# A lag of three pairs in the second MLP: three buffers for h, and both second products of a pair behind seven block products in one go

## The reference, cut to what matters

```python
x = moe_ref(attention(q, k, v))                    # 4608 x 512
h = x @ w_in                                       # 512 -> 1024
e = np.exp(h - h.max(-1)); sm = e / (e.sum(-1) + 1e-9)
solu = h * sm
mu = solu.mean(-1); var = ((solu - mu) ** 2).mean(-1)
ln = (solu - mu) / np.sqrt(var + 1e-6) * g_ln
out = ln @ w_out                                   # 1024 -> 512
```

## Time and profile before

| | |
|---|---|
| time before, median of 3 runs | 1238.48 us (1237.42 to 1242.6) |
| the profiled execution's own time | 1237.77 us |
| its span, first to last instruction | 1236.0 us |
| mean granted TensorE clock | 0.988 |
| PE, DVE, ACT, POOL busy | 97%, 74%, 43%, 25% |
| first block product of the second MLP | starts at 832.63 us |
| copy of the last output tile (ACT, L1163) | starts at 1232.00 us |

### The profile page before, as it was taken

One profiled execution on the slowest core, in us unless ns is written; L12 is line 12 of the kernel. 1 busy time (PEld: TensorE's weight loads), 2 busy tenths in 40 slices (PEclk: granted clock), 3 DMA queues, 4 the chain that ended last, 5 costly groups with the idle time before them and its releaser, 6 DMA issues.

```text
span 1236.0 us, 16164 instructions
## 1 busy us (share of the span) xinstructions
PE 1196.8 (97%) x6013; PEld 988.3 (80%) x6013; DVE 909.0 (74%) x1165; ACT 537.1 (43%) x744; POOL 310.0 (25%) x233
## 2 busy tenths in 40 slices
PE   7999999999999999999999999997889999999997
PEld 6778887878788888888888888985667888888886
DVE  7869678686773577869777686754789888888872
ACT  4443434434353334444434444333454554545441
POOL 5632413224141000000000000124543545353400
PEclk9999999999999999999999999998899999999999
DMA  9797787878865654270642704693355454544333
GB/s 229 226 283 261 238 258 232 249 249 261 268 191 181 236 198 172 74 237 35 196 145 85 238 17 161 207 293 105 125 166 171 150 156 155 152 159 151 135 128 111
DMA packets 211918, 225.07 MB, mean 182 GB/s; under 512 B 63208, under 2 KB 148224, under 8 KB 211712
## 3 DMA queue, kind: packets, MB, share of 16 engines
q1 hardware_dynamic: 206064, 212.50, 54.7%
q0 software_dynamic: 5728, 11.53, 3.3%
q10 hardware_dynamic: 48, 0.01, 0.0%
HBM read 128.51 MB, written 95.48 MB: 181 GB/s over the span
## 4 chain that ended last, share of the span: by engine, by line
PE 77%; DVE 8%; DMA 4%; issue 4%; POOL 2%; SPq 2%; ACT 2%; POOLq 0%; DVEq 0%; ACTq 0%
PE ps_y L1840 8%; PE ps_y L1842 7%; PE ps_y L1841 7%; PE ps_y L1926 5%; PE ps_y L1928 5%; PE ps_y L1930 5%; PE ps_y L1984 5%; PE ps_y L1985 5%; PE ps_y L1986 5%; PE ps_m L1926 3%; PE ps_m L1928 3%; PE ps_m L1930 2%; PE ps_m L1965 2%; PE ps_m L1969 2%; PE ps_m L1967 2%
## 5 line engine op out<-in xcount | busy, mean ns | idle before, releaser
L1840 PE MATMUL ps_y<-X,W 128*128 128x512 f32 x576 | 226.7, 394 | 0.0
L1842 PE MATMUL ps_y<-X,W 128*128 128x512 f32 x576 | 224.4, 390 | 0.0
L1841 PE MATMUL ps_y<-X,W 128*128 128x512 f32 x576 | 224.3, 389 | 0.0
L1364 DVE SCALAR_TENSOR_TENSOR gst<-gst,nslope,ps_y 128x512 f32<-128x512 f32 x144 | 104.4, 732 | 111.0 <-ACT gst L967 110.6
L967 ACT ACTIVATE gst<-ps_y 128x512 f32<-128x512 f32 x144 | 85.7, 596 | 224.8 <-PE ps_y L1842 166.1
L836 POOL TENSOR_TENSOR x2r<-x2r 128x256 f32<-128x256 f32 x18 | 25.1, 1394 | 410.0 <-DMA x2r<-x_scratch 410.0
L1984 PE MATMUL ps_y<-WO,zh 128*128 128x512 f32 x288 | 115.3, 400 | 11.9 <-DVE zl L1665 11.9
L1840 PEld LDWEIGHTS ps_y<-X,W 128*128 128x128 f32 x576 | 108.1, 188 | 23.1
L1842 PEld LDWEIGHTS ps_y<-X,W 128*128 128x128 f32 x576 | 108.1, 188 | 22.8
L1841 PEld LDWEIGHTS ps_y<-X,W 128*128 128x128 f32 x576 | 108.1, 188 | 22.0
L1926 PE MATMUL ps_y<-rh,WOc 128*128 128x512 f32 (+1 forms) x320 | 118.6, 371 | 3.0 <-DVE rl L1526 2.9
(11 more groups left out here) (189 smaller groups left out, 2519.5 us busy)
## 6 DMA issues: line engine op xcount, KB each, us to landing
g_scratch<-gst SPq DMA_DIRECT2D x144, 256.0 KB, 3.5
RX<-g_scratch SPq DMA_DIRECT2D x36, 512.0 KB, 3.6
z_scratch<-zb SPq DMA_DIRECT2D x36, 512.0 KB, 2.7
zt<-z_scratch SPq DMA_DIRECT2D x144, 128.0 KB, 2.9
ws_scratch<-whl SPq DMA_DIRECT2D x22, 512.0 KB, 4.5
RY<-g_scratch SPq DMA_DIRECT2D x18, 512.0 KB, 4.0
RZ<-g_scratch SPq DMA_DIRECT2D x18, 512.0 KB, 4.6
x2r<-x_scratch SPq DMA_DIRECT2D x18, 512.0 KB, 5.0
```

The lines of the kernel that those rows point to most:

```text
L1364: nc.vector.scalar_tensor_tensor(gst[:, n % 3, :], gst[:, n % 3, :], nslope[:, f:f + 1], ps_y[:, f % 4, :], ALU.mult, ALU.add).then_inc(g_ ...
L1840: nc.tensor.matmul(o, W1[:, f, 0, a, :], x[:, 0, a, :], start=(a == 0), stop=False)
L1841: nc.tensor.matmul(o, W1[:, f, 0, a, :], x[:, 1, a, :], start=False, stop=False)
L1842: mm = nc.tensor.matmul(o, W1[:, f, 1, a, :], x[:, 0, a, :], start=False, stop=(a == KT - 1))
```

## The change

PE now does, for pair n, k = 0, 1, 2, 3, 4, 6, 5 in one go and then both tiles of pair n-3. h gets a third buffer. The orders of DVE, ACT, POOL and SP are rewritten to fit. In the last (small) double chunk of the stage before, the units use three buffers instead of two, `x2_high(0)` comes two products earlier, `x2_high(1)` goes between the last two units, `load_x2(1)` is issued earlier (its place in memory is swapped with that of a low part), and DVE does its two posts before the low part of unit (4, 1). The computation is the same. In the two long loops of ACT and DVE below, the conditions that leave out pairs before 0 and behind 17 are not printed.

```diff
-        hs = ((h00, h01), (h10, h11t))
+        hs = ((h00, h01), (h10, h11t), (h20, h21))
...
-                self.slot = 1 + s % 2 if self.single else r % 3
-                if self.single:
-                    self.before = r - 2 if s >= 2 else r - 3
-                else:
-                    self.before = r - 3
+                self.slot = r % 3
+                self.before = r - 3
...
+                if u == PAIRS:                      # SP
+                    sp.wait_ge(bl_ok, number(PAIRS, 3, 1) + 1)
+                    load_x2(1)
                 store_x2(u, 3, p1, c22_ok, 2 * (u + 1), y22_st)
...
+            for n in range(5, PERIODS + 4):         # SP
+                if n - 4 < PERIODS:
+                    store_out(n - 4, 1)
+                if n - 2 < PERIODS:
+                    store_z(n - 2, 0)
+                    load_z(n - 2, 0)
+                if n - 3 < PERIODS:
+                    store_out(n - 3, 0)
+                if n - 2 < PERIODS:
+                    store_z(n - 2, 1)
+                    load_z(n - 2, 1)
                 if n + 3 < PERIODS:
                     load_x2(n + 3)
...
             x2_low(0)                               # POOL
+            x2_sums(1)
             load_wo2(0)
             load_wo2(1)
-            x2_sums(1)
             x2_low(1)
             x2_sums(2)
             x2_low(2)
+            x2_sums(3)
             power(0, 0)
-            x2_sums(3)
             x2_low(3)
+            x2_sums(4)
             power(0, 1)
-            x2_sums(4)
+            x2_low(4)
+            x2_sums(5)
             power(1, 0)
-            x2_low(4)
             power(1, 1)
-            x2_sums(5)
+            x2_low(5)
+            x2_sums(6)
             power(2, 0)
             power(2, 1)
...
+            for n in range(5, PERIODS + 2):
+                power(n - 2, 0)
+                power(n - 2, 1)
                 if n + 1 < PERIODS:
                     x2_low(n + 1)
                 if n + 2 < PERIODS:
                     x2_sums(n + 2)
...
-                    if t.u == LAST_U and t.k == 4:  # ACT, in the units
+                    if t.u == LAST_U and t.k == 2:
                         x2_high(0)
+                if t.u == LAST_U and t.k == 6 and t.j == 0:
+                    x2_high(1)
...
+            for n in range(5, PERIODS + 4):         # ACT; each call only where its pair exists
+                square_tile(n - 2, 1)
+                first_copy(n)
+                out_copy(n - 4, 1)
+                zt_high(n - 3, 1)
+                x2_high(n + 1)
+                out_copy(n - 3, 0)
+                h11_copy(n)
+                zt_high(n - 2, 0)
+                exp_tile(n - 1, 0)
+                exp_tile(n - 1, 1)
+                square_tile(n - 1, 0)
...
+                if t.u == LAST_U and t.k == 4:      # DVE, in the units
+                    if t.j == 0:
+                        post("v", t.u)
+                        post("c22", t.u)
+                    continue
+                if t.u == LAST_U and t.k == 5:
+                    b_turn(UNITS[number(t.u, 4, t.j)])
...
             tile_solu(0, 0)                         # DVE, the single calls
             form_early(1)
+            norm_tile(0, 0)
+            form_21(1)
+            form_12(1)
+            form_early(2)
             tile_solu(0, 1)
...
+            for n in range(5, PERIODS + 3):         # DVE; each call only where its pair exists
+                zt_low(n - 3, 0)
+                form_early(n)
+                form_21(n)
+                form_12(n)
+                norm_tile(n - 2, 0)
+                zt_low(n - 3, 1)
+                norm_tile(n - 2, 1)
+                tile_max(n - 1, 0)
+                tile_max(n - 1, 1)
+                tile_solu(n - 1, 0)
+                tile_solu(n - 1, 1)
...
             for n in range(PERIODS):                # PE
-                for k in range(4):
+                for k in (0, 1, 2, 3, 4, 6, 5):
                     m1_product(n, k)
                 if n >= 3:
+                    m2_product(n - 3, 0)
                     m2_product(n - 3, 1)
-                for k in range(4, PARTS):
-                    m1_product(n, k)
-                if n >= 2:
-                    m2_product(n - 2, 0)
-            m2_product(PERIODS - 3, 1)
-            for n in range(PERIODS - 2, PERIODS):
+            for n in range(PERIODS - 3, PERIODS):
                 for t in range(2):
                     m2_product(n, t)
```

More of the change, by code:

```diff
@@ L713, in _ @@
             load_z(0, 1)
+            load_x2(6)
             store_out(0, 0)
@@ L718, in _ @@
             load_z(1, 1)
-            load_x2(6)
+            load_x2(7)
             store_out(0, 1)
@@ L1168, in _ @@
             exp_tile(0, 0)
+            x2_high(2)
             first_copy(1)
             exp_tile(0, 1)
-            x2_high(2)
             square_tile(0, 0)
             h11_copy(1)
-            square_tile(0, 1)
+            x2_high(3)
             first_copy(2)
-            x2_high(3)
-            exp_tile(1, 0)
             h11_copy(2)
             zt_high(0, 0)
+            square_tile(0, 1)
+            first_copy(3)
+            x2_high(4)
+            exp_tile(1, 0)
             exp_tile(1, 1)
+            zt_high(0, 1)
@@ L1181, in _ @@
             square_tile(1, 0)
-            zt_high(0, 1)
             square_tile(1, 1)
-            first_copy(3)
+            h11_copy(3)
             out_copy(0, 0)
-            x2_high(4)
+            x2_high(5)
             exp_tile(2, 0)
+            first_copy(4)
+            zt_high(1, 0)
             exp_tile(2, 1)
-            zt_high(1, 0)
             out_copy(0, 1)
             square_tile(2, 0)
-            h11_copy(3)
+            zt_high(1, 1)
             square_tile(2, 1)
-            zt_high(1, 1)
+            out_copy(1, 0)
@@ L1195, in _ @@
+            h11_copy(4)
             exp_tile(3, 0)
-            first_copy(4)
-            out_copy(1, 0)
             exp_tile(3, 1)
-            x2_high(5)
+            zt_high(2, 0)
             square_tile(3, 0)
[L1201 to L1213, removed]
+            for n in range(5, PERIODS + 4):
+                if n - 2 < PERIODS:
+                    square_tile(n - 2, 1)
+                if n < PERIODS:
+                    first_copy(n)
+                if n - 4 < PERIODS:
+                    out_copy(n - 4, 1)
+                if n - 3 < PERIODS:
+                    zt_high(n - 3, 1)
@@ L1673, in _ @@
             form_early(0)
+            form_21(0)
             form_12(0)
             tile_max(0, 0)
-            form_21(0)
             tile_max(0, 1)
@@ L1679, in _ @@
             form_early(1)
+            norm_tile(0, 0)
+            form_21(1)
+            form_12(1)
+            form_early(2)
             tile_solu(0, 1)
-            form_12(1)
-            form_21(1)
-            norm_tile(0, 0)
+            zt_low(0, 0)
+            form_21(2)
+            form_12(2)
+            norm_tile(0, 1)
+            form_early(3)
             tile_max(1, 0)
-            form_early(2)
-            norm_tile(0, 1)
-            zt_low(0, 0)
             tile_max(1, 1)
@@ L1689, in _ @@
             tile_solu(1, 0)
-            form_12(2)
-            form_21(2)
             tile_solu(1, 1)
+            zt_low(0, 1)
+            norm_tile(1, 0)
+            form_21(3)
+            form_12(3)
+            norm_tile(1, 1)
             tile_max(2, 0)
             tile_max(2, 1)
-            zt_low(0, 1)
-            norm_tile(1, 0)
-            form_early(3)
-            norm_tile(1, 1)
             tile_solu(2, 0)
             zt_low(1, 0)
+            form_early(4)
             tile_solu(2, 1)
-            form_12(3)
@@ L1703, in _ @@
-            form_21(3)
-            tile_max(3, 0)
             norm_tile(2, 0)
-            tile_max(3, 1)
             norm_tile(2, 1)
             zt_low(1, 1)
+            form_21(4)
+            form_12(4)
+            tile_max(3, 0)
+            tile_max(3, 1)
             tile_solu(3, 0)
-            form_early(4)
             tile_solu(3, 1)
-            norm_tile(3, 0)
-            zt_low(2, 0)
-            form_12(4)
-            form_21(4)
-            tile_max(4, 0)
-            norm_tile(3, 1)
@@ L1718, in _ @@
-            zt_low(2, 1)
-            tile_max(4, 1)
-            tile_solu(4, 0)
-            tile_solu(4, 1)
-            for n in range(5, PERIODS):
-                norm_tile(n - 1, 0)
-                norm_tile(n - 1, 1)
-                form_early(n)
-                zt_low(n - 2, 0)
-                zt_low(n - 2, 1)
-                form_12(n)
-                tile_max(n, 0)
-                form_21(n)
-                tile_max(n, 1)
-                tile_solu(n, 0)
-                tile_solu(n, 1)
@@ L1734, in _ @@
-            n = PERIODS - 1
-            norm_tile(n, 0)
-            norm_tile(n, 1)
-            for t in range(2):
-                zt_low(n - 1, t)
-            for t in range(2):
-                zt_low(n, t)
```

(17 more changed lines are left out.)

109 lines of the change are left out of this document (31 added, 78 removed).

## The result

Predicted were 1277 us (1253 to 1290), with 0.89 for slower. The changed kernel takes a median of 1283.14 us (1278.21 to 1286.8, 4 executions) beside 1237.95 us (1235.4 to 1242.6, 4 executions) for the kernel before: ratio 1.0358, 95% interval 1.0307 to 1.0409. The profiled execution is the fastest of the four, 1278.21 us with a span of 1276.4 us. One execution, of 3055.63 us in experiment 2, was disturbed and is left out of every median and ratio. Every kernel in this study does the whole computation.

What follows compares the result with a forecast made beforehand. The prediction took PE at full clock to bound the middle, with time to win only at the ends. Its terms 926.2 + 286.8 + 57.8 + 4.3 gave a span of 1275.1, forecast 1277.5 us, range 1253 to 1290.

Steps and rivals of the forecast that it cites:

- first block product: Start of the second MLP, where the units end: forecast 833.2 us, against 832.6 before, with some 3.6 idle.
- start of pair 5: Forecast 916.7 us, from work and 14.1 us of stalls in the first pairs; a gain of 13.
- twelve periods: Middle, pair 5 to pair 17: 23.9 us per pair, 286.8 in all (276 to 296); PE alone 244.8.
- the end, up to PE's last matmul: Eight tiles after the last block product: 43.5 us plus waits for low parts and clock, 57.8 (48 to 62).
- Chain A: Middle: POOL's x2_low holds DVE's norm, 3.75 us lost per pair; first_copy late, PE idles 2.6 us per pair.
- X: Moment PE ends the seven products of pair n; first_copy(n+1) is due 16.3 us later.
- R1: Rival: Chain A doesn't happen, Chain B does; period 22.2 to 22.7 us, 1256 us, with clock up to 1265; chance 0.20.
- Chain B: Middle, on ACT: exp stands behind zt_high, which waits for a tile's way through DRAM; late by 1.8 to 2.3 us.
- R2: Rival: neither chain late, PE stays the bound; 1232 us, or 1223 with a shorter end; chance 0.11.
- The clock: PE's clock falling behind gaps, 1.7 us lost each; in the middle taken for half of the pairs.
- from the execution to the median: Last step of the sum: 0.7 us added, as the median before was above its profiled execution; 1276.9 to 1277.5.
- The stalls up to pair 5 and at the end: Idle in units 3.6, pair 2 5.2, pair 4 2.4 and 1.9, tile (1, 1) 0.7; end 6.6 and 3.3 us.

Runs made afterwards that it cites:

- experiment 2: Changed kernel with both exp ahead of zt_high(n-2, 0) on ACT: 1274.18 us, ratio 1.0287 against the kernel before.
- experiment 1: Changed kernel with POOL's x2_low(n) waiting until both tiles of pair n-3 are past the norm: 1283.24 us, ratio 1.0365 against the kernel before.
- experiment 3: Changed kernel with both edits, x2_low waiting for the norm and exp ahead of zt_high: 1231.93 us, ratio 0.995 against the kernel before.
- experiment 4: Changed kernel with exp ahead of zt_high and, from pair 6, POOL's x2_low cut into two 128x896 instructions: 1247.03 us, ratio 1.0066.
- experiment 7: Kernel of experiment 6 with zt_low(n, 0) of pairs 15 and 16 between the two solu of the pair behind: 1233.78 us, ratio 0.9962.
- experiment 6: Kernel of experiment 3 with norm_tile(0, 0) moved behind form_21(1) and form_12(1) on DVE: 1234.58 us, ratio 0.9974 against the kernel before.
- experiment 5: Kernel before with only the units' part of the change, second MLP as before: 1228.89 us, ratio 0.9923.

## Why the prediction was right

Its sum, term by term, against the profiled execution of the changed kernel:

| term | predicted | measured |
|---|---|---|
| first block product | 833.2 | 833.56 |
| start of pair 5 | 916.7 | 916.66 |
| end of its block products | 926.2 | 916.66 + 42 x 0.2267 = 926.2 |
| twelve periods | 286.8 | 1213.09 - 926.2 = 286.9 |
| the end, up to PE's last matmul | 57.8 | 1272.26 - 1213.09 = 59.2 |
| last output | 4.3 | 1276.4 - 1272.26 = 4.1 |
| span | 1275.1 | 1276.4 |

PE's last matmul starts at 1272.03; with the 0.23 us that one takes from start to start, that is 1272.26.

The first row is close partly by luck. Six more profiled executions have the same code up to there; in those of experiments 1 to 4 and 7 the first block product starts at 834.37 to 836.65, in that of experiment 6, behind one more stall, at 840.22.

**Chain A** was the chain that decides. Predicted: L1656 (L1639 now) at 4.3 to 4.6 us in some 13 instructions, POOL 0.06 ahead of it, the copy at X + 18.9, gaps of 2.6. Measured: 4.53, 13, 0.07, X + 19.0, 2.73. Experiment 4 shows the cause by its size, and experiments 2 and 3 by its presence. Rival R1's mechanism is out: POOL was first in all 13 meetings, by 0.06 to 0.07 us. The Trainium skill (SBUF — State Buffer, section "SBUF: two separate sides") has the lock held for the whole instruction; experiment 4 agrees, 2.60 us behind half of POOL's instruction and 4.53 behind all of it.

**Chain B** was there, covered by A. Experiment 1 uncovers it with 2.11 us, of which some 0.3 is a solu that met POOL's sums (1.60 instead of 1.28). Its middle is R1's case too, and R1 was priced too low: it gave 22.4 us a period and 1256 in all, and the twelve periods of experiment 1 take 1217.0 - 929.2 = 287.8, which is 24.0 each. That sum left out the edge of each gap and the clock. So the time could not have told A from B; the held norm and the length of the gap did.

**R2** asked for both chains to be in time and gave 1232. The kernel of experiment 3 is that case, at 1231.93. The middle is as R2 had it (244.7 us for 244.8), but the two ends only cancel: pair 5's block products end at 928.7 and not 923, and what follows the last block product is 57.4 us and not 62.1.

**The clock** is the term whose parts were off. I had taken half of the twelve pairs at 1.7 us; it was 4 pairs at 1.4. What filled the sum up again was the edge of a gap, 0.3 us each, and a gap longer by 0.1: 23.44 for the predicted 23.0 with full clock, 24.85 for 24.7 without. The sum of 286.8 is right partly by that luck, and only in this execution. Another execution of the same kernel took 8.6 us more, at a mean clock of 0.976.

**The stalls up to pair 5 and at the end.** Predicted and measured idle time: units 3.6 and 3.35; k = 1 of pair 2 5.2 and 4.84; in pair 4 2.4 and 2.19, 1.9 and 1.50; tile (1, 1) 0.7 and 1.37. At the end, 6.6 and 6.56, 3.3 and 3.72, and one of 0.68 that I had not seen. The clock behind them was put at 2.7 and 0.8 up to pair 5 and at 2.7 and 1.6 at the end; the rows ahead of the prediction show only 1.7, behind 2.34 us, and no working leads from there to these terms. The window up to the end of pair 5's block products is:

```profile
833.56:926.20 92.64, 82.56 (x351) 65.91 (x350) 65.37 (x102) 40.80 (x58) 34.41 (x30) 0.98 0.43 137
```

A clock of 0.98 over 92.64 us is some 1.9 us lost, where 3.5 had been put. The edges of the gaps, which the sum lacked, fill most of that.

**The step that was off** is the last one, from the execution to the median. I added the 0.7 us by which the kernel before differed. The median of the changed kernel is 4.9 above its profiled execution. The mean clock of the four executions was 0.984, 0.976, 0.986 and 0.981, so the profile is one draw of several, and the fastest. The clock is not all of it, as the execution at 0.986 took 2.5 us more than the one at 0.984. That step makes 4.2 of the 5.6 us between the 1277.5 of the sum and the 1283.14 measured.

**Where the change's gain is.** It won 18.5 us up to the start of pair 5 (916.66 against 935.14), of which 5.4 is the tile not yet done. Of the other 13, 7.3 are the part about the units, by experiment 5, which leaves some 6 for the new order of the first pairs; in the trace of experiment 3 pair 5 starts at 919.15, and it is 3. The lag has nothing to win in the middle, where PE was already the bound, and as ordered here it brings two late chains there; mended (experiment 3), it is not faster than the kernel without it (3 us behind in the median).

**What stays open.** Why the clock falls behind some gaps and not others can't be told from these rows: gaps of 2.73 us lost it every third time in the changed kernel's trace and in no such order in experiment 2's, 7 of 12. So it is also not shown that the shorter gaps of experiment 1 cost more clock; that may be the draw. The head of experiment 3 is not solved either: two stalls of 2 to 5 us remain in the first pairs, and one reordering only moved the larger. A combination of the kernel before with a better tail was not tried.

## What to carry to other kernels

Where the bound engine is free of gaps, a new order can win only at the two ends; work out the due time of each thing it waits for in the middle, since half a microsecond per period decides the sign. When two chains are late side by side, mending one shows little (0 and some 9 us here, 51 together): uncover the second before the first is acquitted. A long operation on GpSimd directly behind a small one that VectorE waits for started first and held VectorE's in all 13 meetings here; place it behind VectorE's operation by a semaphore, or cut it up.

## What the runs showed of the hardware

The granted clock behind a gap is not a function of the gap's length alone. Behind gaps of 2.73 us it fell in 4 of 12 pairs in one execution and in 7 of 12 in another (experiment 2), behind gaps of 2.1 us in 7 of 10 (experiment 1), behind 0.85 us in none of 12 (experiment 4). Six microseconds less of idle time bought nothing where the gaps stayed above 2 us. The spread between executions is not explained by the gaps alone: 8.6 us for the changed kernel and 0.8 for that with gaps of 0.85, but 7.2 for the kernel before, which has none in the middle.

VectorE's one-input L1639, held by POOL, ended 0.55 us behind POOL's end rather than its full 0.81. Cutting POOL's instruction in two cost 0.6 us on POOL (4.65 for 4.05) and gave VectorE 1.93 us back (2.60 for 4.53).
